# Pooling keys from 8 KB rows: six wide loads, a 128x32 pooling product, and the coefficient loads moved behind the weights

## The reference, cut to what is computed

```python
# q: (1, 12288, 128); kv: (1, 384, 32, 128); w_sr: (128, 128)
kv_pool = kv.reshape(B, H // 4, 4, W // 4, 4, C).mean(axis=(2, 4))   # 96 x 8 cells of 4x4 pixels
k = v = kv_pool.reshape(B, -1, C) @ w_sr                             # 768 keys
s = scale * (q @ k.transpose(0, 2, 1))
x = softmax(s) @ v                                                   # 12288 tokens
h = x @ w_in; g = max(h, 0) + alpha * min(h, 0); x = g @ w_out       # first layer, d_ff 2048
h = x @ w_in2; g = P(h) / (Q(|h|) + 1e-6); out = g @ w_out2          # second layer, cubic P, quadratic Q
```

## Time and profile before

| | us |
|---|---|
| median of three runs | 1563.15 |
| lowest and highest | 1561.4, 1563.31 |
| the profiled execution | 1564.52 |
| its span, first to last instruction | 1562.7 |

### The profile page before, as it was taken

One profiled execution on the slowest core, in us unless ns is written; L12 is line 12 of the kernel. 1 busy time (PEld: TensorE's weight loads), 2 busy tenths in 40 slices (PEclk: granted clock), 3 DMA queues, 4 the chain that ended last, 5 costly groups with the idle time before them and its releaser, 6 DMA issues. The chain is left out here.

```text
span 1562.7 us, 28287 instructions
## 1 busy us (share of the span) xinstructions
PE 1509.7 (97%) x8269; PEld 1242.8 (80%) x8269; DVE 1432.4 (92%) x2257; ACT 1401.7 (90%) x2714; POOL 1237.9 (79%) x1352
## 2 busy tenths in 40 slices
PE   5999999979999999999999999999999999999986
PEld 5899999846788888888888888888888888888865
DVE  4788888727999999999999999999999999999997
ACT  1777777637999999999999999999999999999996
POOL 0444444405999999999999999999999999999998
PEclk9999999999999999999999999999999999999998
DMA  8110110000000000000000000000000000000000
GB/s 244 48 28 22 28 48 21 1 0 1 8 1 8 8 8 8 2 8 8 8 1 8 8 8 8 1 8 8 8 8 1 8 8 8 1 8 8 8 8 8
DMA packets 12330, 24.94 MB, mean 16 GB/s; under 512 B 1536, under 2 KB 1680, under 8 KB 11920
## 3 DMA queue, kind: packets, MB, share of 16 engines
q1 hardware_dynamic: 11424, 22.55, 4.8%
q10 hardware_dynamic: 752, 0.60, 0.1%
HBM read 16.85 MB, written 6.29 MB: 15 GB/s over the span
## 5 line engine op out<-in xcount | busy, mean ns | idle before, releaser
L270 POOL TENSOR_TENSOR cubic<-sq,lin_p 128x512 f32<-128x512 f32 x384 | 495.6, 1291 | 84.3 <-ACT sq L458 59.7
L261 POOL TENSOR_TENSOR rational<-newton,ratio 128x512 f32<-128x512 f32 x336 | 434.0, 1292 | 29.5 <-PE banks L1073 21.2
L1073 PEld LDWEIGHTS banks<-wout,rational 128*128 128x128 f32 x3072 | 399.8, 192 | 44.0 <-issue 11.0
L880 PE MATMUL banks<-x_hi,win_lo 128*128 128x512 f32 x768 | 387.1, 504 | 25.6 <-DVE ratio L747 13.5
L1073 PE MATMUL banks<-wout,rational 128*128 128x128 f32 x3072 | 402.7, 276 | 3.8 <-POOL rational L261 3.8
L882 PE MATMUL banks<-x_hi,win_hi 128*128 128x512 f32 x768 | 303.4, 395 | 0.0
L881 PE MATMUL banks<-x_lo,win_hi 128*128 128x512 f32 x768 | 302.9, 394 | 0.0
L476 ACT ACTIVATE lin_p<-banks,ab_raw 128x512 f32<-128x512 f32 x384 | 298.4, 777 | 1.0 <-PE banks L882 1.0
L730 DVE SCALAR_TENSOR_TENSOR banks<-sq,abs_b,banks 128x512 f32<-128x512 f32 x384 | 286.9, 747 | 2.9 <-ACT banks L468 2.5
L738 DVE SCALAR_TENSOR_TENSOR banks<-banks,ab_raw,cubic 128x512 f32<-128x512 f32 x384 | 288.3, 751 | 0.8 <-POOL cubic L270 0.8
L747 DVE SCALAR_TENSOR_TENSOR ratio<-banks,ab_raw,rcp 128x512 f32<-128x512 f32 x384 | 285.7, 744 | 1.8
(11 more groups left out here) (91 smaller groups left out, 2261.3 us busy)
## 6 DMA issues: line engine op xcount, KB each, us to landing
early<-in_kv_dram SPq DMA_DIRECT2D x24, 256.0 KB, 10.1
out_dram<-y_out SPq DMA_DIRECT2D x24, 256.0 KB, 2.0
neg_part<-in_q_dram SPq DMA_DIRECT2D x22, 256.0 KB, 2.7
early<-in_moe_w_in_dram SPq DMA_DIRECT2D x1, 1024.0 KB, 16.4
wout<-in_moe_w_in_dram SPq DMA_DIRECT2D x1, 1024.0 KB, 5.2
neg_part<-in_q_dram ACTq DMA_DIRECT2D x2, 256.0 KB, 9.3
early<-in_w_sr_dram ACTq DMA_DIRECT2D x1, 64.0 KB, 1.9
wout<-in_moe_w_out_dram SPq DMA_DIRECT2D x2, 0.5 KB, 12.6
```

What stands on the lines that cost most here:

```text
L261: nc.gpsimd.tensor_tensor(rational[:, m % 3, :], newton[:, m % 2, :], ratio[:, m % 2, :], ALU.mult).then_inc(s["rat_done"], 1)
L270: nc.gpsimd.tensor_tensor(cubic[:, m % 2, :], sq[:, m % 2, :], lin_p[:, m % 2, :], ALU.mult).then_inc(s["cubic_done"], 1)
L880: nc.tensor.matmul(dst, w[1], x[0], start=start, stop=False)
L1073: last = nc.tensor.matmul(banks[:, ACC2, t * P:(t + 1) * P], rational[:, m % 3, t * P:(t + 1) * P], wout2[:, c, :], start=(c == 0 and t == ...
```

## The change

kv is read as rows of 8 KB. An image row (32 pixels x 128 channels, 16 KB) is cut in two halves; chunk (k, n) takes 128 image rows, one for each partition, and half n of each. So a partition holds 16 pixels of one image row: four runs (UNITS = 4) of four neighbours. There are seven transfers in place of 24: five of 1 MB, and the last chunk in two of 512 KB, with a semaphore each.

Pooling over the four neighbours of a run is done within a partition, and pooling over four image rows is done across partitions, by a product with `row_sums`, a 128x32 matrix of ones made from the identity by one DVE reduction. A unit (one run of one chunk) is pooled by PE alone with four such products, or by a DVE reduction of 512 elements to 128 and one product. DVE takes 3, 2, 2, 3, 2, 2 units of the six chunks, 14 of 24. The two coefficient loads move from ACT's queue, ahead of q, to SP's queue, behind w_out1. The absolute values of b move from ACT's start to behind `wout1_hi`, and the waits for them from ahead of `one_minus_al` to ahead of `wout1_lo`.

```diff
-    kv_rows = kv[0].rearrange("(hh r) (ww x) c -> hh ww r (x c)", r=POOL_SIDE, x=POOL_SIDE)
+    kv_rows = kv[0].rearrange("(k h) (n w) c -> k n h (w c)", h=P, n=2)
+    CELLS = P // POOL_SIDE
+    UNITS = P // CELLS
...
+        BY_DVE_UNITS = ((0, 1, 2), (0, 1), (0, 1), (0, 1, 2), (0, 1), (0, 2))
...
-            for c in range(CHUNKS):
-                for r in range(POOL_SIDE):
-                    sp.dma_start(kv_in[:, c, r * POOL_SIDE * P:(r + 1) * POOL_SIDE * P],
-                                 kv_rows[c * key_rows:(c + 1) * key_rows, :, r, :]).then_inc(s[f"ld_kv{c}{'aabb'[r]}"], 16)
+            for c in range(CHUNKS - 1):
+                sp.dma_start(kv_in[:, c, :], kv_rows[c // 2, c % 2]).then_inc(s[f"ld_kv{c}"], 16)
+            half = UNITS // 2 * POOL_SIDE * P
+            sp.dma_start(kv_in[:, CHUNKS - 1, 0:half], kv_rows[CHUNKS // 2 - 1, 1, :, 0:half]).then_inc(s[f"ld_kv{CHUNKS - 1}"], 16)
+            sp.dma_start(kv_in[:, CHUNKS - 1, half:], kv_rows[CHUNKS // 2 - 1, 1, :, half:]).then_inc(s["ld_kv_rest"], 16)
             sp.dma_start(raw_in[0], w_in1).then_inc(s["ld_in1"], 16)
             sp.dma_start(wout1[:], w_out1.rearrange("(b p) c -> p b c", p=P)).then_inc(s["ld_out1"], 16)
+            sp.dma_start(ab_raw[:, 0:4], coef_p.partition_broadcast(P)).then_inc(s["ld_ab"], 16)
+            sp.dma_start(ab_raw[:, 4:6], coef_q.partition_broadcast(P)).then_inc(s["ld_ab"], 16)
...
-            act.dma_start(ab_raw[:, 0:4], coef_p.partition_broadcast(P)).then_inc(s["ld_ab"], 16)
-            act.dma_start(ab_raw[:, 4:6], coef_q.partition_broadcast(P)).then_inc(s["ld_ab"], 16)
...
-            act.wait_ge(s["ld_ab"], 32)
-            nc.scalar.activation(abs_b[:], ab_raw[:, 4:6], ACT.Abs).then_inc(s["absb_col_done"], 1)
...
-            act.wait_ge(s["cols_done"], 1)
+            act.wait_ge(s["ld_ab"], 32)
+            nc.scalar.activation(abs_b[:], ab_raw[:, 4:6], ACT.Abs).then_inc(s["absb_col_done"], 1)
+            act.wait_ge(s["absb_col_done"], 1)
...
-                dve.wait_ge(s[f"ld_kv{c}a"], 32)
-                nc.vector.tensor_reduce(pooled[:, c, :],
-                                        kv_in[:, c, 0:DVE_PIXELS * P].rearrange("p (j c) -> p c j", j=DVE_PIXELS),
-                                        AX.X, ALU.add).then_inc(s["pooled_done"], 1)
+                dve.wait_ge(s[f"ld_kv{c}"], 16)
+                for u in BY_DVE_UNITS[c]:
+                    if c == CHUNKS - 1 and u >= UNITS // 2:
+                        dve.wait_ge(s["ld_kv_rest"], 16)
+                    pixels = kv_in[:, c, u * POOL_SIDE * P:(u + 1) * POOL_SIDE * P]
+                    nc.vector.tensor_reduce(pooled[:, c, u, :], pixels.rearrange("p (x n) -> p n x", x=POOL_SIDE),
+                                            AX.X, ALU.add).then_inc(s["pooled_done"], 1)
...
-            dve.wait_ge(s["ld_ab"], 32)
-            dve.wait_ge(s["absb_col_done"], 1)
             dve.wait_ge(s["al_ready"], 1)
...
+            dve.wait_ge(s["ld_ab"], 32)
+            dve.wait_ge(s["absb_col_done"], 1)
             dve.wait_ge(s["out1_hi_done"], 1)
...
-                pe.wait_ge(s[f"ld_kv{c}b"], 32)
-                for j in range(DVE_PIXELS, PIXELS):
-                    nc.tensor.matmul(dst, kv_in[:, c, j * P:(j + 1) * P], ident[:], start=(j == DVE_PIXELS), stop=False)
-                pe.wait_ge(s["pooled_done"], c + 1)
-                nc.tensor.matmul(dst, pooled[:, c, :], ident[:], start=False, stop=True).then_inc(s["pooled_t_ready"], 1)
+                pe.wait_ge(s[f"ld_kv{c}"], 16)
...
+                for u in by_pe:
+                    if c == CHUNKS - 1 and u >= UNITS // 2:
+                        pe.wait_ge(s["ld_kv_rest"], 16)
+                    for x in range(POOL_SIDE):
+                        at = (u * POOL_SIDE + x) * P
+                        nc.tensor.matmul(banks[:, POOLED[c], u * CELLS:(u + 1) * CELLS], kv_in[:, c, at:at + P], row_sums,
+                                         start=(u == by_pe[0] and x == 0), stop=False, skip_group_check=True)
+                for n, u in enumerate(BY_DVE_UNITS[c]):
+                    pe.wait_ge(s["pooled_done"], made_before + n + 1)
+                    last = nc.tensor.matmul(banks[:, POOLED[c], u * CELLS:(u + 1) * CELLS], pooled[:, c, u, :], row_sums,
+                                            start=False, stop=(n == len(BY_DVE_UNITS[c]) - 1), skip_group_check=True)
+                last.then_inc(s["pooled_t_ready"], 1)
```

More of the change, by code:

```diff
@@ L43, in build @@
     assert d == P and BLOCKS == 16 and TILES == 4 and CHUNKS == 6 and GROUPS % 6 == 0
-    kv_rows = kv[0].rearrange("(hh r) (ww x) c -> hh ww r (x c)", r=POOL_SIDE, x=POOL_SIDE)
-    key_rows = P // kv_rows.shape[1]
+    kv_rows = kv[0].rearrange("(k h) (n w) c -> k n h (w c)", h=P, n=2)
+    CELLS = P // POOL_SIDE
+    UNITS = P // CELLS
     q_groups = q[0].rearrange("(g p t) c -> g p (t c)", p=P, t=TILES)
@@ L99, in build @@
         w_in1_t = early[:, tokens // 2 + ff:tokens // 2 + 2 * ff].rearrange("p (b c) -> p b c", b=BLOCKS)
-        pooled = early[:, 0:keys].rearrange("p (c n) -> p c n", c=CHUNKS)
-        w_sr_sb = early[:, keys:keys + P]
-        al_rows = early[0:BLOCKS, keys + P:keys + 2 * P]
+        w_sr_sb = early[:, 0:P]
+        al_rows = early[0:BLOCKS, P:2 * P]
+        row_sums = early[:, 2 * P:2 * P + CELLS]
+        pooled = early[:, 3 * P:3 * P + CHUNKS * UNITS * P].rearrange("p (c u n) -> p c u n", c=CHUNKS, u=UNITS)
         q_in = neg_part
@@ L111, in scores @@
             return banks[:, 2 * n:2 * n + 2, 0:HALF]
-        DVE_PIXELS, POOLED, VALUES = 2 * POOL_SIDE, (2, 3, 5, 6, 7, 2), (3, 6)
+        BY_DVE_UNITS = ((0, 1, 2), (0, 1), (0, 1), (0, 1, 2), (0, 1), (0, 2))
+        POOLED, VALUES = (2, 3, 5, 6, 7, 2), (3, 6)
         Q_T, P_T, ATT = 4, (5, 6), 7
@@ L119, in build @@
         for name in (
-            *(f"ld_kv{c}{part}" for c in range(CHUNKS) for part in "ab"), "ld_wsr", "ld_in1", "ld_out1", "ld_in2", "ld_out2", "ld_al", "ld_ab", "ld_q0", "ld_q1", "st_out",
+            *(f"ld_kv{c}" for c in range(CHUNKS)), "ld_kv_rest", "row_sums_done", "ld_wsr", "ld_in1", "ld_out1", "ld_in2", "ld_out2", "ld_al", "ld_ab", "ld_q0", "ld_q1", "st_out",
             "ident0", "absb_col_done", "al_ready", "ident_ready", "pooled_done", "pooled_t_ready", "pooled_t_copied", "k_ready", "k_hi_done", "k_lo_done",
@@ L635, in scale_out1 @@
                                         ALU.mult).then_inc(s["out1_scaled"], 1)
+            dve.wait_ge(s["ident_ready"], 1)
+            nc.vector.tensor_reduce(row_sums, ident[:].rearrange("p (n r) -> p n r", r=POOL_SIDE),
+                                    AX.X, ALU.add).then_inc(s["row_sums_done"], 1)
             pool_keys(0)
-            dve.wait_ge(s["ld_ab"], 32)
-            dve.wait_ge(s["absb_col_done"], 1)
             dve.wait_ge(s["al_ready"], 1)
@@ L889, in pooled_transpose @@
             def pooled_transpose(c):
-                dst = banks[:, POOLED[c], 0:P]
+                by_pe = [u for u in range(UNITS) if u not in BY_DVE_UNITS[c]]
+                made_before = sum(len(units) for units in BY_DVE_UNITS[:c])
                 if c == 4:
@@ L895, in pooled_transpose @@
                     pe.wait_ge(s["pooled_t_copied"], 1)
-                pe.wait_ge(s[f"ld_kv{c}b"], 32)
-                for j in range(DVE_PIXELS, PIXELS):
-                    nc.tensor.matmul(dst, kv_in[:, c, j * P:(j + 1) * P], ident[:], start=(j == DVE_PIXELS), stop=False)
-                pe.wait_ge(s["pooled_done"], c + 1)
-                nc.tensor.matmul(dst, pooled[:, c, :], ident[:], start=False, stop=True).then_inc(s["pooled_t_ready"], 1)
+                pe.wait_ge(s[f"ld_kv{c}"], 16)
+                if c == 0:
+                    pe.wait_ge(s["row_sums_done"], 1)
+                for u in by_pe:
[10 more added lines that the diff above has]
+                last.then_inc(s["pooled_t_ready"], 1)
             def key_chunk(c):
```

## The result

The changed kernel takes 1564.86 us (median of 21 runs, 1563.27 to 1566.92) against 1562.15 us for the kernel before beside it (1559.87 to 1565.45): ratio 1.0016, 95% interval 1.0009 to 1.0023. It is slower by 2.7 us by the medians (2.5 by the ratio), where 10 us of gain were forecast. Its profiled execution took 1565.45 us, its span 1563.7 us; the profiled execution of before stood 2.4 us above that kernel's median, so the spans understate the difference and the stages are better read one by one.

What follows compares the result with a forecast made beforehand. Waiting for kv was taken to bound the load phase. Last DVE unit 23.8 + 0.45 + 2.03 = 26.3 us against 36.39; 10.1 gained less 0.15 for the passage gives 1553.2 us, range 1549.5 to 1558.5 (own range 1550.5 to 1555.5).

Steps and rivals of the forecast that it cites:

- What bounds the kernel before: Load phase: no compute engine is the limit, DVE and PE wait for kv, and time saved there moves everything behind forward.
- The transfers: kv loads: 8 KB rows raise 279 GB/s to 392, so kv takes 16.1 us in place of 22.5.
- rival (b): kv loads: the rate stays near 279 GB/s; gain 2.5 to 4 us, time 1560 us; chance 9%.
- DVE: Pooling: 14 reductions of 0.95 us, 13.3 us in all; DVE, not the transfer, is last by 1.8 us.
- rival (a): Pooling on DVE: half-size reductions cost 1.2 to 1.5 us; gain 4 to 7 us, time 1557.5 us; chance 12%.
- PE, the step that failed: Pooling on PE: a 10-product chunk takes at most 2.5 us, under the chunk's 2.7, so it costs the path nothing.
- rival (c): TensorE idles between chunks and enters the scores at 1.2 GHz; up to 3 us lost, 1556.2 us; chance 9%.
- What is late next: Loads behind kv: w_in1 and group 2 of q arrive in time, q's group by 2 to 4 us.
- the passage: Attention to expert stage: the moved absolute values put 0.1 to 0.25 us onto the path, taken as 0.15.
- The sum: First score at 26.3 us against 36.39, 10.1 us gained; net 10.0 us, time 1553.2 us.
- Rival (d): kv loads: new rows run below 226 GB/s and the phase ends later; 1567 us at 200 GB/s; chance 3%.
- rival (e): A late q or weight load takes gain back: 2 to 4 us lost, 1556 us; chance 6%.

Runs made afterwards that it cites:

- second experiment: Changed kernel with 22 products of the identity with itself ahead of the first kv product, pooling products still 32 columns: 1562.5 us, ratio to before 0.999.
- first experiment: Changed kernel with every pooling product streaming 128 columns in place of 32, padded with zeros: 1554.35 us, ratio to before 0.994.
- last experiment: Changed kernel with 128-column pooling products and 11 products of the identity with itself ahead of the first kv product: 1554.38 us, ratio to before 0.9946.

## Why the prediction was wrong, point by point

- **What bounds the kernel before**: right. Taking the transfers' hole away alone brought the first score 2.7 us forward and the median down by 1.9 us.
- **The transfers**: 392 GB/s forecast, 419 measured, so rival (b) is out; the first chunk forecast for 6.6 us, and DVE's first reduction began at 6.25. The size was right, but its attribution to 8 KB rows was for the most part wrong: the 2 KB runs of the new layout ran at 378 to 403. The hole that I gave nothing, and 2 us at most, was worth 2.7 us in the kernel before.
- **DVE**: its price was right. Three reductions took 2.89 us, five 4.76, so 0.95 to 0.96 each against 0.95 forecast, and rival (a) is out. That the strided read sets this time was not tested. That DVE would be the last engine was wrong, as the next point says.
- **PE, the step that failed.** I priced the pooling records at the spacing of a warm TensorE and concluded that PE "costs the path nothing" at either end of the bounds. The upper bound was not an upper bound. The row of the first chunk at half clock was in front of me, and 140 records at 0.214 us are 29.9 us, more than all of DVE's work. I used that row only for rival (c), and there priced a cold clock at the last chunk and the scores (up to 3 us), not over the whole pooling, where it cost 10 (the 9.9 us between the changed kernel and its 128-column version at the first score). Rival (c) had the right clock for the wrong reason: it feared idle time between the chunks, and the clock stayed low in a PE that was never idle. The list of rivals had none that made PE the bound of the phase; only the last sign of being wrong, "matmul spacings doubled past 25 us", names what came. I also gave 32 columns a price between that of 128 and near nothing. Sixteen records took 1.87 against 1.95 us at 2.4 GHz, and in the first chunk, at 1.2 GHz, eight took 1.91 against 2.08.
- **Two readings in the prediction.** 421 and 281 ns are durations of overlapping records and stand as 1.5 to 1; the spacing by the starts is 0.218 to 0.118 us. And a gain of 8 us with 1 us of spread gives 1556.2 us as the upper end of the forecast's own range, not 1555.5. Neither bears on the step that failed.
- **By the Trainium skill** (TensorE: Matmul & The Clock Gate, Part 1, the HAM clock gate) half rate is the default and activity releases it; I read activity as "not idle". The second experiment shows 0.50 in a stretch with PE busy 10.00 of 10.00 us, so the busy time of these rows is not what holds the clock up. How wide a product must be was not tried between 32 and 128 columns.
- **By the same page of the Trainium skill** (section LDWEIGHTS) loading the stationary operand takes a time set by its columns. Every pooling product here loads 128 of them. The weight loads in the traces agree: their mean time is the same for 32 as for 128 streamed columns, 333 and 331 ns at half clock (changed kernel from 26 to 30 us, 128-column version from 7 to 13 us), 192 ns for both at full clock (second and first experiment, 14 to 17 us). That bears on a spacing that hardly falls with the streamed columns; no run here varied the weights' columns, so that they set the spacing is argued, not shown.
- **What is late next, the passage**: right. Neither w_in1 nor group 2 of q was waited for, and the passage lost 0.20 us in the changed kernel, 0.15 in the experiments, as forecast.
- **The sum**: with the one step mended by wide products, the first score came at 27.38 against 26.3 forecast and the time was 1554.35 against 1553.2. That it came so near is in part luck: the forecast's path ends with DVE, which was done at 23.52 (23.8 forecast), but PE came 1.2 us after it, and the rest took 2.64 us in place of 2.48. The step on PE is thus wrong at full clock too, by 1.2 us: from 19.61 on PE never waited, with the keys' and values' products and two whole chunks still to do, 0.11 us a record. The half-clock start up to 13 us is already inside these times of DVE and PE; without it, in the last experiment, both came 0.9 us earlier.

Rival (d), slower through slow transfers, had the right sign by the wrong mechanism, and rival (e), the gain taken back by a late load, did not occur.

## What to carry to other kernels

Price matmuls at both clocks before calling them free: if a change makes products narrower, or removes columns while the number of products stays, multiply all records of the stage by the half-clock spacing of the trace and see whether PE becomes the bound. Padding the moving operand with zeros to 128 columns was the better of the two mends tried here: four times the columns, 10.5 us less (wide products ahead of narrow ones: 2.4 us less). And a TensorE that is busy in every stretch is no sign of full clock: read records per microsecond (4.9 against some 10 at full clock here).

## What the hardware showed that was not expected

- TensorE's clock fell to 0.50 under uninterrupted, mostly narrow f32 products, 16 records in 3.46 us (second experiment). In the changed kernel it rose 3 us after 384-column products began (score at 40.31), in the other runs that entered the scores at half clock 1.1 to 2.4 us after.
- In the kernel before, with 128 columns, it held though PE idled for 2.0 of 10 us (20 to 30 us): sixteen records still took 2.05 us.
- The column of the granted clock reads 1.00 from the start of each of these traces to the first fall that it shows, at either clock: in the changed kernel it says 1.00 from 30 to 40 us with records 0.214 us apart. The spacing of records has to decide there.
- Two broadcasts of 2 KB and 1 KB to 128 partitions, issued beside the bulk load, took the rate of all transfers to 47 GB/s for a microsecond and cost 2.7 us at the first score.
- Two layouts with 2 KB runs differ, from 10 to 20 us, as 266 to 310 GB/s (the kernel before and its two variants) to 378 to 403: with sixteen pixels of a cell from four image rows spread over transfers, and with one image row for each partition. What in the addresses makes the difference was not tried.
